# GpSimd's early pieces in other steps, and no identity matmuls in the first two steps, in an attention and gated-MLP kernel

## The reference

```python
scores = scale * q @ k.T + bias(relu(psi * w1 + b1) @ w2)
attn = exp(scores - max(scores)); attn = attn / (sum(attn) + 1e-09)
x = (attn @ v) laid out as [tokens, 512]
out = (sigmoid(x @ w_gate) * (x @ w_val)) @ w_out
```

## The kernel before

| pair | m = 0 | m = 1 | m = 2 | m = 3 | R |
| --- | --- | --- | --- | --- | --- |
| 9 | | | S1 | | S1 |
| 10 | S2, S2 | S3 | S3 | | S4 |
| 11 | S4, low A11 | low A11 | low A12 | | low A12 |
| 12 | low A22, A22 | low S1 | low S1 | | low S2 |
| 13 | low S2, weight sum 0 | weight sum 1 | low S3 | | low S3 |
| 14 | low S4, S4 | weight sum 2 | low B1 | | |
| 15 | low TA | low TB | | | |

## Time and profile before

### The profile page before, as it was taken

How to read it: one execution, slowest core, us unless ns; L and a number is a source line. 1 busy time by engine, 2 the same in 40 slices (tenths; PEclk the granted TensorE clock), 3 DMA queues, 4 the chain that set the end, 5 groups by cost and what they waited for, 6 DMA issues and landing times.

```text
span 735.9 us, 14243 instructions
## 1 busy us (share of the span) xinstructions
PE 714.7 (97%) x4962; PEld 588.1 (80%) x4962; DVE 507.7 (69%) x1065; ACT 463.9 (63%) x934; POOL 354.1 (48%) x473
## 2 busy tenths in 40 slices
PE   7779999999999999999999999999999999999998
PEld 4337777677777666789889998998899899989997
DVE  7996777777777888738814868784178758705841
ACT  7998777777778777767516752763367437516720
POOL 0004555554569898755564625562155355504500
PEclk9999999999999999999999999999999999999999
DMA  6886232222362222133310241211022422201002
GB/s 178 217 207 149 65 104 75 68 67 76 98 230 75 67 67 69 42 102 127 118 42 30 86 143 72 73 58 58 1 78 67 158 73 68 76 0 58 30 10 76
DMA packets 56886, 63.64 MB, mean 86 GB/s; under 512 B 22128, under 2 KB 48240, under 8 KB 56816
## 3 DMA queue, kind: packets, MB, share of 16 engines
q1 hardware_dynamic: 56384, 62.65, 28.6%
q10 hardware_dynamic: 432, 0.09, 0.1%
HBM read 42.67 MB, written 9.44 MB: 71 GB/s over the span
## 4 chain that ended last, share of the span: by engine, by line
PE 82%; DVE 11%; issue 3%; ACT 2%; DMA 1%; POOL 0%; ACTq 0%; DVEq 0%; POOLq 0%
PE f_ps L1372 20%; PE z_ps L1303 19%; PE v_ps L1265 10%; PE y_ps L1303 10%; DVE feats L936 7%; PE so_ps L1211 7%; PE x_ps L1303 5%; PE ty_ps L1222 4%; PE tx_ps L1232 3%; PE so_ps L1206 2%; PE tx_ps L1245 1%; ACT probs L754 1%; DVE sum_eps L976 1%; DVE neg_scores L961 1%; PE tx_ps L1235 1%
## 5 line engine op out<-in xcount | busy, mean ns | idle before, releaser
L1303 PE MATMUL z_ps<-xc,wc 128*128 128x384 f32 x864 | 165.5, 336 | 0.6 <-DVE wc L1018 0.5
L1303 PEld LDWEIGHTS z_ps<-xc,wc 128*128 128x128 f32 x864 | 150.5, 188 | 4.0 <-ACT keep L781 1.6
L754 ACT ACTIVATE probs<-neg_scores,neg_max 128x576 f32<-128x576 f32 x144 | 110.8, 770 | 46.0 <-DVE neg_max L961 45.6
L586 POOL TENSOR_SCALAR probs<-probs,recip 128x512 f32<-128x512 f32 x144 | 99.0, 699 | 79.5 <-DVE recip L981 79.5
L961 DVE CUSTOM_DVE_ANT_0 neg_scores<-so_ps,bias 128x576 f32<-128x576 f32 x128 | 92.2, 755 | 5.3 <-PE so_ps L1194 3.9
L613 POOL TENSOR_TENSOR wc<-t_raw,wc 128x512 fp32r<-128x512 f32 x37 | 48.8, 1318 | 87.6 <-ACT wc L773 87.6
L1303 PE MATMUL y_ps<-xc,wc 128*128 128x384 f32 x432 | 86.6, 334 | 0.5 <-DVE sig L1034 0.5
L781 ACT ACTIVATE keep<-z_ps 128x384 f32<-128x384 f32 x108 | 52.9, 490 | 52.3 <-PE z_ps L1303 51.7
L1372 PE MATMUL f_ps<-wo_h,h_h 128*128 128x512 f32 x210 | 82.1, 391 | 0.7 <-issue 0.7
L599 POOL TENSOR_TENSOR t_raw<-w_stage 128x512 f32<-128x512 f32 x36 | 50.4, 1399 | 66.2 <-DVE wc L1018 66.2
L1372 PE MATMUL f_ps<-wo_h,h_l 128*128 128x512 f32 x210 | 82.0, 391 | 0.0
(11 more groups left out here) (125 smaller groups left out, 1427.0 us busy)
## 6 DMA issues: line engine op xcount, KB each, us to landing
qk_whole<-in_qk SPq DMA_DIRECT2D x16, 608.0 KB, 4.7
w_stage<-in_w_gate SPq DMA_DIRECT2D x18, 512.0 KB, 3.5
w_stage<-in_w_val SPq DMA_DIRECT2D x18, 512.0 KB, 3.6
bias<-bias_rows SPq DMA_DIRECT2D x12, 576.0 KB, 5.1
out<-out_sb SPq DMA_DIRECT2D x17, 256.0 KB, 2.0
v_main<-in_v SPq DMA_DIRECT2D x32, 128.0 KB, 2.3
x_whole<-attn_transposed SPq DMA_DIRECT2D x9, 384.0 KB, 6.0
wo_whole<-in_w_out SPq DMA_DIRECT2D x6, 512.0 KB, 4.6
```

The source lines that it names most:

```text
L586: nc.gpsimd.tensor_scalar(row, row, recip[:, stat(s, place)], 1.0, ALU.mult, ALU.mult).then_inc(normed, 1)
L754: nc.scalar.activation(probs[s % RING][:, place, :], neg_scores[:, shift_place(s, place), :], ACT.Exp, bias=neg_max[:, stat(s, place)], sc ...
L1303: last = nc.tensor.matmul(quad_ps[bank][n % 2][:, 0:CH], wc[:, n % 2, wl, W_PARTS.index(wp), t, :], xc[:, X_PARTS.index(x), xl, t, :], sta ...
```

## The change

FILLERS and the loop that used it are deleted. The table of pieces is a dict by (pair, m): the same pieces, but none behind the third step (m = 2) and one behind the fourth (m = 3) in pairs 9 to 14. In pair 10 nothing is left behind m = 1. The kinds change places a little in pairs 13 and 14: all three weight sums are in pair 13 (m = 1, m = 3, R), B1 is behind (14, 1), and the low parts of S3 and S4 are in pair 14. Pair 15 and B22 are as before.

```diff
--- before.py
+++ after.py
@@ -34,7 +34,6 @@
 TAIL_LWIN = TAIL_LAST_BASE + S
 ROW_BUFS = 4
 WARM_UP = 6
-FILLERS = 3
 PREP_UNIT = 6
 
 QK_UNITS = (7, 11)
@@ -310,15 +309,24 @@
         X_LOAD_AT = SPP * (2 * HP + 1)
 
 
-        TASK_STEPS = [X_LOAD_AT + 2, X_LOAD_AT + R]
-        TASK_STEPS += [pair * SPP + m for pair in range(2 * HP + 2, PAIRS) for m in (0, 0, 1, 2, R)]
-        PIECES = [("x", "sum", k, n) for k in ("S1", "S2", "S3", "S4") for n in range(KH)]
-        PIECES += [("x", "low", k, n) for k in ("A11", "A12", "A22", "S1", "S2") for n in range(KH)]
-        PIECES += [("w", "sum", n) for n in range(2)]
-        PIECES += [("x", "low", "S3", n) for n in range(KH)] + [("x", "low", "S4", n) for n in range(KH)]
-        PIECES += [("w", "sum", 2), ("w", "low", "B1"), None, ("w", "low", "TA"), None, ("w", "low", "TB"), None, None]
-        PIECES += [("w", "low", "B22")]
-        TASKS = [(s, piece) for s, piece in zip(TASK_STEPS + [STEPS], PIECES) if piece]
+        def x_lows(k):
+            return [("x", "low", k, n) for n in range(KH)]
+
+        def x_sums(k):
+            return [("x", "sum", k, n) for n in range(KH)]
+
+        def w_low(g):
+            return [("w", "low", g)]
+
+        W_SUMS = [("w", "sum", n) for n in range(3)]
+        TASKS = {(9, 3): x_sums("S1")[:1], (9, R): x_sums("S1")[1:],
+                 (10, 0): x_sums("S2"), (10, 3): x_sums("S3")[:1], (10, R): x_sums("S3")[1:],
+                 (11, 0): x_sums("S4"), (11, 1): x_lows("A11")[:1], (11, 3): x_lows("A11")[1:], (11, R): x_lows("A12")[:1],
+                 (12, 0): x_lows("A12")[1:] + x_lows("A22")[:1], (12, 1): x_lows("A22")[1:],
+                 (12, 3): x_lows("S1")[:1], (12, R): x_lows("S1")[1:],
+                 (13, 0): x_lows("S2"), (13, 1): W_SUMS[:1], (13, 3): W_SUMS[1:2], (13, R): W_SUMS[2:],
+                 (14, 0): x_lows("S3"), (14, 1): w_low("B1"), (14, 3): x_lows("S4")[:1], (14, R): x_lows("S4")[1:],
+                 (15, 0): w_low("TA"), (15, 1): w_low("TB"), (16, 0): w_low("B22")}
         HIGH_STEPS = [pair * SPP + m for pair in range(2 * HP + 2, PAIRS) for m in (0, R)]
         HIGHS = {s: k for s, k in zip(HIGH_STEPS, ("A11", "A12", "A22", "S1", "S2", None, "S3", "S4",
                                                    "B1", "TA", "TB", "B22")) if k}
@@ -652,9 +660,8 @@
                     if s % SPP != R:
                         for u, place in units_of(s):
                             normalise_tails(s, place)
-                for at, (of, *piece) in TASKS:
-                    if at == s:
-                        (first_x if of == "x" else first_w)(*piece)
+                for of, *piece in TASKS.get(divmod(s, SPP), ()):
+                    (first_x if of == "x" else first_w)(*piece)
 
             def low_x(c, k):
                 pool.wait_ge(x_high[k], c + 1)
@@ -1314,10 +1321,6 @@
                 c = s - LAG
                 if s < STEPS:
                     scores(s)
-                if s < 2:
-
-                    for n in range(FILLERS):
-                        nc.tensor.matmul(v_ps[:, 0:P + REM], ident, ident_wide[:, :], start=True, stop=True)
                 if m in VALUES_FIRST and pair >= 1:
                     values(pair - 1, *VALUE_SLOTS[m])
                 if 0 <= c < STEPS and c % SPP == R:
```

## The result

| | before | after |
| --- | --- | --- |
| median of the runs | 737.82 us (6 runs) | 742.47 us (6 runs, 741.7 to 743.01) |
| profiled execution, span | 735.9 us | 741.2 us |
| granted TensorE clock, mean | 1.000 | 0.993 |
| first values matmul of pair 1 | 75.10 | 78.40 |
| first values matmul behind pair 15 | 313.46 | 318.73 |

The kernel became slower: ratio 1.0057, interval [1.0046, 1.0069], 4.65 us. 739.8 was forecast with a range up to 741.6; the median lies 0.9 us above that range. Single executions of one kernel at a mean clock of 1.000 lie at two levels, for the kernel before about 737.6 and about 739.0; what sets them apart is not known, so differences under a microsecond are not read from single executions here. The spans of the two profiled executions differ by 5.3. Of that, 3.30 is there before pair 1 starts, and 5.27 when the last pair is over.

The account below looks back on a forecast made before the run. Attention was taken as bound by TensorE. Identity matmuls at 0 and pieces at 0, 0.48, 0.48, 0.52, 0.35 and 0.26, together 2.1 us, on a median of 737.66 gave 739.8, range 735.6 to 741.6.

Parts of the forecast that it names:

- The pieces: Attention pairs 10 to 15: the later R piece holds line 976 of step 0, delaying R's scores; 2.1 us slower.
- The identity's time: Attention steps 0 and 1: removing 2.48 us of identity matmuls gains 0, covered by the last bias store; bounds 0 and -2.5.
- The clock: Rival at the start of attention: without identity matmuls TensorE falls to 1.2 GHz for steps 2 to 4; 743, chance 0.06.

Follow-up runs that it names:

- the run with 64 rows: The kernel before with its identity matmuls in steps 0 and 1 using 64 rows of the array instead of 128: 737.72 us, ratio 1.0001.

## Why the prediction failed

**The pieces: right.** The step was worked out as line 976 of step 0 held by an R piece that comes 0.99 later, passed on through GpSimd and VectorE to the scores of R, 0.48 a pair and 2.1 us in all. Measured: 1.96 us in the pairs of the changed kernel; as the new table alone 1.9 in the pairs and 1.7 by the medians. The terms were 0, 0.48, 0.48, 0.52, 0.35 and 0.26 for pairs 10 to 15; they measured -0.13, 0.37, 0.39, 0.63, 0.55 and 0.15. The 0.48 is 0.1 too high since I started it from pair 12 of before, where the tails ended late because of the piece at m = 2 that the change takes away: the new piece begins at 252.97 - 251.89 = 1.08, not 1.17. In pairs 13 and 14 the 128x512 piece at m = 1 was taken at 1.74, the length of one that met a shorter operation of VectorE; its row after is 1.93 in both:

```profile
278.75 1.93 POOL L607 TENSOR_TENSOR t_raw<-w_stage 128x512 f32<-128x512 f32 x1
...
295.28 1.93 POOL L621 TENSOR_TENSOR wc<-w_stage,wc 128x512 fp32r<-128x512 f32 x1
```

That it all goes through line 976 was argued from three ends that agreed to 0.03; the two kernels without that line show it.

**The identity's time: right.** It was priced at nothing because the last bias store covers it. The shift of step 2 stayed at 67.76, the one execution of the deletion alone that kept its clock took 738.06, and one identity matmul per step instead of three changes nothing beyond the interval.

**The clock: this step failed.** The sum counted the deletion as 0, for the time of the matmuls alone, and left the clock out as a rival with a chance of 0.06. The ground for that chance was that the stretch of 18 to 24 us had TensorE busy in 4.03 of 6 us at a clock of 1.00 and the stretch of 62 to 68 would have 3.5. The row is read rightly, but neither the estimate nor the conclusion held. TensorE was busy in 5.3 of the 6 us from 62 to 68 in the changed kernel. Part of that is that the scores of step 1 alone take 1.92 us without the identity (62.72 to 64.64) where they took 1.37 (63.95 to 65.32): with it, some matmuls of one head run beside those of the other (in step 1 two of them start at 64.32 and 64.33). And at this busier stretch the clock fell, while at 4.03 of 6 it had held, so the busy share did not tell. What the runs showed in place of the 0 is 1.5 us in the median for the deletion alone, and 3.1 to 3.3 us in executions at a mean clock of 0.993. The price of the rival, 743, was near the 742.47 measured, and its mechanism was the right one; its chance was not.

The Trainium skill (TensorE: Matmul & The Clock Gate, Part 1), which I set aside with the remark that every gap is broken by matmuls, has the fall after idle time. In two of the three traces with a fall TensorE had waited shortly before, but only 0.67 and 0.66 us; in the trace of the deletion alone it fell after more than 5 us without a break. There the trace does not agree with the Trainium skill, and the measurement decides.

Of the 4.65 us, then, 1.7 to 1.9 are the pieces and the rest is TensorE at 1.2 GHz: next to nothing in an execution that keeps its clock, 3.1 to 3.4 at a mean clock of 0.993. The three traces with a fall have it for 3.4, 6.8 and 10.2 us, at mean clocks of 0.998, 0.995 and 0.993. How often and how long it falls differs from execution to execution (median clocks of 0.994 in both sets of the changed kernel, 0.995 for the deletion alone). The sum of the two parts by the medians, 3.2, is less than the 4.65 and 4.25 measured; that the difference is only which executions were drawn fits the comparison at one clock, but is not shown further.

**Open:** what in the stretch without the identity brings the clock down. It is not a wait of TensorE just before, at least not in the deletion alone. Two things are left. In the changed kernel the scores of the two heads in steps 0 and 1 run one after the other, without a matmul of another kind between them from 60.8 on. But with the identity behind step 1 alone that row is there too, up to the first identity matmul at 64.60, and the clock held in 11 of 11; the deletion alone fell at 65.0, less than half a microsecond later. And each of those scores uses only half of the rows of the array; whether that matters the run with 64 rows leaves open, as said there.

## What to carry to other kernels

Work that seems to do nothing, on an engine whose clock is granted, may be there for the clock: before taking it out, try it alone and look at the clock in several single executions; how busy the engine would be did not tell it here. Then try how little of it is enough. For small work in the gaps of another engine, find the one instruction that is held by it, and place the pieces by when that instruction arrives; or write that instruction in a form that is not held.

## What was not expected of the hardware

- The clock fell to 1.2 GHz at 65.0 us in a stretch where TensorE issued score matmuls without a gap, and stayed down for 6.8 us; in one profile of the changed kernel it was down for 10.2, in the other for 3.4. Without identity matmuls it held in 1 of 11 executions with the old table and in 1 of 12 with the new one. One (two instructions, 0.5 us) in each of two steps went with a full clock in 11 of 11 executions; three in step 0 alone in 9 of 12.
- A two-column tensor_scalar of VectorE is held by a GpSimd tensor_tensor to the very end of it (1.06 instead of 0.17), and if it arrives in the last 0.08 us of one piece with another right behind, through that one too. A reciprocal of the same shape is not held (0.17 in the middle of a piece); in the three traces without line 976 all that began inside a piece took 0.16 to 0.17. The Trainium skill (SBUF — State Buffer, Who interferes with whom) names tensor_scalar among the operations that can take the shared ports; the reciprocal is not in its list, and the runs show it free.
- Adding epsilon to the denominator was expensive for what it does: leaving it out is worth 3.0 us between the profiled executions and 3.4 between the medians, of 737.9.
